# Routing and scattering each 96-token chunk inside a batch-major attention loop, with one region of rows per expert

## The reference, cut to what matters

```python
def _moe_ref(x, w_gate, w1, w2, capacity):
    logits = x @ w_gate
    expert_idx = np.argmax(logits, axis=1)
...
    for i in range(N):
        e = expert_idx[i]
        if counts[e] < capacity:
            disp[e, counts[e]] = x[i]
            pos[i] = counts[e]
            counts[e] += 1
            keep[i] = True
    h = np.maximum(np.einsum('ecd,edf->ecf', disp, w1), 0.0)
    y = np.einsum('ecf,efd->ecd', h, w2)
...
    for i in range(N):
        if keep[i]:
            out[i] = gate_w[i] * y[expert_idx[i], pos[i]]
def _moe2_ref(x, w_a, w_b, w_out):
    a = x @ w_a
    b = x @ w_b
    return (a * b @ w_out).astype(np.float32)
```

## Time and profile before

| what | value |
|---|---|
| runs | 677.47, 677.79, 680.08 us; median 677.79 us |
| span of the profiled execution, first to last instruction | 679.2 us |
| its own device time | not given apart from its span; its span lies inside the three times |
| TensorE busy | 511.9 us, 75% |
| VectorE busy | 381.5 us, 56% |
| ScalarE busy | 263.2 us, 39% |
| POOL busy | 39.9 us, 6% |
| mean granted TensorE clock | 0.958 of full speed |
| DMA | 60.5 MB, 89 GB/s on average |

### The profile page before, as it was taken

How to read it: one execution, slowest core, us unless ns; L and a number is a source line. 1 busy time by engine, 2 the same in 40 slices (tenths; PEclk the granted TensorE clock), 3 DMA queues, 4 the chain that set the end, 5 groups by cost and what they waited for, 6 DMA issues and landing times.

```text
span 679.2 us, 9804 instructions
## 1 busy us (share of the span) xinstructions
PE 511.9 (75%) x3682; PEld 475.1 (70%) x3683; DVE 381.5 (56%) x751; ACT 263.2 (39%) x483; POOL 39.9 (6%) x47
## 2 busy tenths in 40 slices
PE   0000001688999994088999999899999999999995
PEld 0000001578999993088999999888888888888884
DVE  3999999997555546245777777644432222221220
ACT  6930514881111113134766667534433121131121
POOL 1000000000000002750000000000002000020002
PEclk9999999789999996588999999989999999999998
DMA  8960001341121105665455554422101000010001
GB/s 335 297 64 0 0 0 69 140 122 37 36 55 36 37 1 204 215 201 198 132 198 185 184 183 140 141 70 92 49 0 47 1 0 1 0 47 0 0 0 46
DMA packets 47955, 60.49 MB, mean 89 GB/s; under 512 B 25072, under 2 KB 40944, under 8 KB 47408
## 3 DMA queue, kind: packets, MB, share of 16 engines
q1 hardware_dynamic: 46384, 55.28, 26.5%
q0 software_dynamic: 1536, 4.73, 2.0%
HBM read 50.55 MB, written 9.45 MB: 88 GB/s over the span
## 4 chain that ended last, share of the span: by engine, by line
PE 70%; DVE 19%; ACT 3%; issue 3%; POOL 3%; DMA 2%; SPq 0%; ACTq 0%; DVEq 0%; POOLq 0%
PE bank L1065 23%; PE bank L1052 10%; PE bank L931 10%; PE bank L895 10%; PE bank L580 4%; PE bank L488 3%; PE bank L559 3%; DVE region L313 3%; DVE XN L310 2%; POOL sorted_x L714 2%; PE bank L584 2%; DVE XN L311 2%; PE bank L595 1%; DVE XN L350 1%; DVE QN L350 1%
## 5 line engine op out<-in xcount | busy, mean ns | idle before, releaser
L1083 DVE TENSOR_TENSOR ga<-ga,bank 128x512 f32<-128x512 f32 x36 | 24.8, 688 | 137.4 <-PE bank L1065 137.4
L366 PE MATMUL bank<-ident,ends 128*96 128x128 f32 x4 | 1.1, 420 | 100.5 <-DVE ends L329 100.5
L366 PEld LDWEIGHTS bank<-ident,ends 128*96 128x96 f32 x4 | 0.6, 187 | 100.1 <-issue 100.1
L931 PE MATMUL bank<-hh,w2h 128*128 128x256 f32 x192 | 54.4, 283 | 1.8 <-ACT w1h L736 1.8
L895 PE MATMUL bank<-xh,w1h 128*128 x192 | 54.4, 284 | 0.0
L931 PE MATMUL bank<-hh,w2l 128*128 128x256 f32 x192 | 54.2, 283 | 0.0
L931 PE MATMUL bank<-hl,w2h 128*128 128x256 f32 x192 | 54.2, 282 | 0.0
L895 PE MATMUL bank<-xh,w1l 128*128 x192 | 53.7, 280 | 0.0
L895 PE MATMUL bank<-xl,w1h 128*128 x192 | 53.6, 279 | 0.0
L1085 ACT ACTIVATE gh<-ga 128x512 fp32r<-128x512 f32 x36 | 22.8, 632 | 79.1 <-DVE ga L1083 79.1
L1081 ACT ACTIVATE ga<-bank 128x512 f32<-128x512 f32 x36 | 21.5, 597 | 80.7 <-PE bank L1065 80.7
(11 more groups left out here) (175 smaller groups left out, 1373.5 us busy)
## 6 DMA issues: line engine op xcount, KB each, us to landing
raw<-w SPq DMA_DIRECT2D x16, 1536.0 KB, 7.1
x_rows<-XN SPq DMA_DIRECT2D x4, 1152.0 KB, 4.2
XN<-x_rows SPq DMA_DIRECT2D x14, 288.0 KB, 3.1
region<-k SPq DMA_DIRECT2D x4, 576.0 KB, 12.6
region<-q SPq DMA_DIRECT2D x4, 576.0 KB, 16.2
V<-v SPq DMA_DIRECT2D x1, 2304.0 KB, 29.3
raw<-wa SPq DMA_DIRECT2D x6, 384.0 KB, 3.2
raw<-wb SPq DMA_DIRECT2D x6, 384.0 KB, 3.9
```

What stands on the lines that cost most here:

```text
L931: m = nc.tensor.matmul(bank[YB0 + c][:, 0:cols], wx[:, f, c * P:(c + 1) * P], xx[:, f, 0:cols], start=f == 0 and i == 0, stop=f == NF - 1 ...
L1083: m = dve.done(tt(ga[f % 2][:], ga[f % 2][:], bb[:, 0:TT], ALU.mult))
```

## The change

The units are now ordered by batch, then piece, then group, and the host hands q, k, v, a_re and a_im over with the two batches swapped, so that the batch worked first is the first half of the tokens. Chunk t of 96 tokens is complete after units 2t and 2t+1, in token order. The diff below is in the order of the streams: the zero fill behind the input loads, ScalarE's wait in front of the copy to eT (L369), three operations more in `set_up`, the loop's new helpers and where it calls them (`choose` ahead of `scores(n + 1)`; `ranks` and `place_chunk` behind u and ahead of y; the wait ahead of the product with `swap`), what follows the loop, and the experts. Each chunk is routed inside the loop: its choice of expert (`choose`), its rank by two or three small products (`ranks`), its slots and its scatter (`place_chunk`). The slot is e x 1536 + rank, in a `sorted_x` with a region of rows for each expert; regions are filled with zeros up to the capacity at the start. w1 and w2 of expert 0 are loaded half way through the loop into memory that QT of the first batch left. Rows are read for one expert at a time (384 rows), and turned and split inside `outputs` of the expert before. Gate and index no longer travel with the rows: after `hidden(0)` VectorE works out the final place of each token and its gate, and POOL scatters pairs (gate, index) to a small DRAM table `place_rows`, which is read back during expert 6.

```diff
+            zero = eT[:, :, :].rearrange("p i q -> p (i q)")[:, 0:DM]
+            m_zrow = pool.done(g.memset(zero, 0.0))
+            sp.wait_ge(pool.sem, m_zrow[1])
+            for e in range(E):
+                sp.dma_start(sorted_x[e, 0:CAP, :].rearrange("(i p) c -> p i c", p=P),
+                             zero.unsqueeze(1).broadcast_to([P, XT_N, DM])).then_inc(s_zero, 16)
...
+            ss.wait_ge(s_zero, 16 * E)
+            m_eT = act.done(ss.activation(eT[0:C2], bank[7][0:C2, :].rearrange("p (i q) -> p i q", i=4), ACT.Copy))
...
+                dve.done(vv.tensor_copy(trib[:], tri[:]))
+                dve.done(vv.tensor_scalar(baseb[:], basef[0:L], ident[0:L, 0:1], None, ALU.mult))
+                m_const.append(dve.done(vv.tensor_copy(mark[:, :, 1], tok)))
...
-            units = [(j, gr) for j in range(NC) for gr in range(NU)]
+            GB = NU // B
+            units = [(j, (B - 1 - b) * GB + gr) for b in range(B) for j in range(NC) for gr in range(GB)]
...
+            def choose(t):
+                dve.wait(m_lgs[t])
+                m = dve.done(vv.tensor_reduce(out=mx[:, t:t + 1], in_=lg(t), axis=AXX, op=ALU.max))
+                dve.wait(m)
+                m = dve.done(vv.scalar_tensor_tensor(out=eqp, in0=lg(t), scalar=mx[:, t:t + 1], in1=pri,
+                                                     op0=ALU.is_equal, op1=ALU.mult))
+                m_read_lg = m
+                dve.wait(m)
+                m = dve.done(vv.tensor_reduce(out=best[:, t:t + 1], in_=eqp, axis=AXX, op=ALU.max))
+                dve.wait(m)
+                m_oh[t] = dve.done(vv.tensor_scalar(ohb[:, t, :], eqp, best[:, t:t + 1], None, ALU.is_equal))
+                act.wait(m_read_lg)
+                m_lx.append(act.done(ss.activation(lgs[:, t, :], lg(t), ACT.Copy)))
+            def ranks(t, m_jd_last):
+                pe.wait(m_oh[t], *m_const)
+                if m_jd_last:
+                    pe.wait(m_jd_last)
+                nc.tensor.matmul(rk[0:L], onesb[:, 0:L], baseb[:], start=True, stop=False)
+                if t:
+                    pe.wait(m_so[t - 1])
+                    nc.tensor.matmul(rk[0:L], onesb[:, 0:L], so[:, t - 1, :], start=False, stop=False)
+                m_rk[t] = pe.done(nc.tensor.matmul(rk[0:L], trib[:], ohb[:, t, :], start=False, stop=True))
+            def place_chunk(t):
+                if t:
+                    dve.wait(m_so[t - 1], m_oh[t])
+                    m_so[t] = dve.done(tt(so[:, t, :], so[:, t - 1, :], ohb[:, t, :], ALU.add))
+                else:
+                    dve.wait(m_oh[0])
+                    m_so[0] = dve.done(vv.tensor_copy(so[:, 0, :], ohb[:, 0, :]))
+                dve.wait(m_rk[t])
+                m_tk[t] = dve.done(tt(sel[:, t, :], rk[0:L], ohb[:, t, :], ALU.mult))
+                dve.wait(m_tk[t])
+                m = dve.done(vv.tensor_reduce(out=rank[:, t:t + 1], in_=sel[:, t, :], axis=AXX, op=ALU.add))
+                dve.wait(m)
+                m_slot[t] = dve.done(vv.tensor_copy(sloti[:, t:t + 1], rank[:, t:t + 1]))
+                pool.wait(m_slot[t], m_yx[(t + 1) * GB - 1])
+                if t == 0:
+                    g.wait_ge(s_zero, 16 * E)
+                g.indirect_dma_start(out=sorted_x.rearrange("e n c -> (e n) c"),
+                                     out_offset=bass.IndirectOffsetOnAxis(ap=sloti[:, t:t + 1], axis=0),
+                                     in_=X[:, t, :], in_offset=None).then_inc(s_sc, 16)
...
+                if n % GB == 1 and done >= 0 and n > GB:
+                    choose(done)
...
+                if n == NUNIT // 2:
+                    sp.wait_ge(pe.sem, m_y[n - 1][1])
+                    for s_, x, y in ((s_w1, w1[0].rearrange("(c p) f -> p c f", p=P), raw_0[0]),
+                                     (s_w2, w2[0].rearrange("(f p) n -> p f n", p=P), raw_0[1])):
+                        sp.dma_start(y.rearrange("p (c f) -> p c f", f=x.shape[-1]), x).then_inc(s_, 16)
...
+                if n % GB == 1 and done >= 0 and n > GB:
+                    ranks(done, m_turned_z)
+                    place_chunk(done)
...
+                        if m_tk:
+                            pe.wait(m_tk[max(m_tk)])
                         m_j = pe.done(nc.tensor.matmul(bank[7][0:C2, 0:YB * D], swap[:], zm[0], start=True, stop=True))
...
+            sp.wait_ge(s_sc, 16 * TAU)
+            load_rows(0)
...
+        for i in range(4):
+            nc.tensor.matmul(bank[i][:, 0:CAP], ident[:], ident[:].unsqueeze(1).broadcast_to([P, XT_N, P]),
+                             start=True, stop=True)
...
+        m_t0 = [turn_tile(i, bank[4 + i]) for i in range(XT_N)]
+        for i in range(XT_N):
+            m_x0 = split_tile(i, bank[4 + i], m_t0[i])
+        sp.wait_ge(pe.sem, m_t0[-1][1])
+        load_rows(1)
...
+                    i = f // 2
+                    if f % 2 and i < tiles:
+                        if i:
+                            pe.wait(m_x[i - 1])
+                        else:
+                            nc.tensor.wait_ge(s_row, (e + 2) * 16)
...
-                w1_marks[0] = [split(*piece1(f)) for f in range(NF)]
+                w1_marks[0] = []
+                for f in range(NF):
+                    w1_marks[0].append(split(*piece1(f)))
+                    if f % 2 and f // 2 < tiles:
+                        assert split_tile(f // 2, bank[7], m_t[f // 2]) == m_x[f // 2]
+                row_marks[0] = (m_t[-1], m_x[-1])
...
+        m_w2 = hidden(0, m_x0, True)
...
+        def chosen(out_, x):
+            D_(tt(sel, ohb[:], over_t(x), ALU.mult))
+            D_(vv.tensor_reduce(out=out_, in_=sel, axis=AXX, op=ALU.add))
...
+        m = D_(tt(ex, lgs, over_e(mx), ALU.subtract))
+        act.wait(m)
+        m_exp = act.done(ss.activation(ex, ex, ACT.Exp))
+        D_(tt(over, tot, kept, ALU.subtract))
+        D_(vv.tensor_tensor_scan(out=cumo, data0=one8, data1=over, initial=cumk[:, E - 1:E],
+                                 op0=ALU.mult, op1=ALU.add))
+        D_(tt(frs, cumo, over, ALU.subtract))
+        D_(vv.scalar_tensor_tensor(out=frs, in0=frs, scalar=-float(CAP), in1=fst, op0=ALU.add,
+                                   op1=ALU.subtract))
+        chosen(comp, basef)
+        D_(tt(rank, rank, comp, ALU.subtract))
+        chosen(comp, frs)
+        D_(vv.scalar_tensor_tensor(out=comp, in0=rank, scalar=float(CAP), in1=comp, op0=ALU.is_ge, op1=ALU.mult))
+        D_(tt(rank, rank, comp, ALU.add))
+        chosen(comp, fst)
+        D_(tt(rank, rank, comp, ALU.add))
+        dve.done(vv.tensor_copy(compi[:], rank))
+        dve.wait(m_exp)
+        D_(vv.tensor_reduce(out=den, in_=ex, axis=AXX, op=ALU.add))
+        D_(vv.tensor_scalar(den, den, 1e-9, None, ALU.add))
+        D_(vv.reciprocal(den, den))
+        m_mark = D_(tt(mark[:, :, 0], den, den, ALU.mult))
+        s_mark, s_placed = sem("s_mark"), sem("s_placed")
+        pool.wait(m_mark)
+        for t in range(TAU):
+            g.indirect_dma_start(out=place_rows[:, :],
+                                 out_offset=bass.IndirectOffsetOnAxis(ap=compi[:, t:t + 1], axis=0),
+                                 in_=mark[:, t, :], in_offset=None).then_inc(s_mark, 16)
...
         def trip(e, more=True):
             outputs(e, False)
+            sp_wait(row_marks[0][0])
+            if more:
+                load_rows(e + 2)
```

More of the change, by code:

```diff
@@ L496, in scores @@
                     SC[r], maski, bank[2 + r][0:L, 0:YB * L].rearrange("p (i c) -> p i c", i=YB)))
+            loaded = [n for n in range(0, len(units), XB) if units[n][0] < NC - 1]
             def load_x(i):
-                j, gr = units[i * XB]
-                if i >= len(XS):
-                    sp.wait_ge(pe.sem, m_u[(i - len(XS) + 1) * XB - 1][1])
-                sp.dma_start(XS[i % len(XS)],
+                j, gr = units[loaded[i]]
+                if i >= NXS:
+                    sp.wait_ge(pe.sem, m_u[loaded[i - NXS] + XB - 1][1])
+                sp.dma_start(XS[i % NXS],
@@ L535, in build @@
+            s_w1, s_w2 = sem("s_w1"), sem("s_w2")
             NUNIT = len(units)
-            NX = (NC - 1) * NU // XB
+            NX = len(loaded)
             sp.wait_ge(s_xrows, 16 * SL)
             sp.wait_ge(pe.sem, m_turn[len(late_q0) + len(late_x) - 1][1])
-            for i in range(len(XS)):
+            for i in range(NXS):
                 load_x(i)
             scores(0)
+            m_added = m_turned_z = None
             for n in range(NUNIT + 2):
+                done, turned, x_at = chunk(n) - 1, None, None
+                if n % GB == 1 and done >= 0 and n > GB:
+                    choose(done)
@@ L543, in build @@
                 if n + 1 < NUNIT:
                     scores(n + 1)
-                turned = None
-                if n - 1 in ready:
+                if n % GB == 0 and n:
+                    turned = chunk(n - 1)
                     pe.wait(m_yx[n - 1])
-                    turned = turn_rows(ready[n - 1], n)
```

(53 more changed lines are left out.)

362 lines of the change are left out of this document (147 added, 215 removed).

## The result

The kernel after the change takes 682.26 us, median of four runs (681.49 to 685.29); the kernel before, run beside it, takes 677.95 us, median of four (677.47 to 680.08). The ratio is 1.0071 with a 95% interval of 1.0044 to 1.0099: slower by 0.4% to 1.0%. The forecast was 663.2 us, 656 to 671, and faster; it was wrong, in size and in sign.

A forecast was written before the change was run, and what follows sets the result against it. TensorE was taken to bound the loop and the experts, with a 52.4 us chain between (258.5 to 310.85 us). Terms 0.5 + 1.8 + 2.0 - 26.2 + 1.4 + 5.9 = -14.6 gave a median of 663.2 us, range 656 to 671.

The forecast's parts named there:

- Points 1 and 2: Start of kernel: zero fill behind the loads, price 0; three more small VectorE operations in set_up, +0.5 us.
- Points 3 and 4: Attention loop: rank products for 15 chunks, +1.8 us; TensorE's waits at three uncovered places, +2.0 us (bounds 0.5 and 5).
- D: Rival, loop: routing chain between VectorE and TensorE becomes each chunk's bound; slower, 682 us; chance 0.05.
- E: Rival, loop: POOL is held, scatters pile up and the last stands behind 15 others; 683 us; chance 0.04.
- Point 5: Last y to outputs(0): 26.2 us instead of 52.4, of which 14.5 until hidden(0) starts; -26.2 us.
- Point 6: outputs(0): a 2.1 us wait behind VectorE's small operations replaces the low clock; 11.5 for 10.08 us, +1.4.
- Point 7: outputs(1) to (6): three tiles in each, 18 x 0.33 us on a full TensorE, +5.9 us.
- Point 8: Experts: 16 small scatters on idle POOL and a 12 KB read in expert 6, long before use; price 0.
- The offset to the median: Whole sum: made against the profiled span, 679.2 us, taken as 1.4 above the 677.8 median, difference carried over.
- A: Rival: clock stays at 1.2 GHz for all of hidden(0) and falls again in outputs(0); 669 us; chance 0.10.
- B: Rival, expert trips: w1 loads start later behind rows and land late, up to 1.5 us in six trips; 672; chance 0.08.
- C: Rival, loop: POOL's scatter holds VectorE as well, 15 x 0.92 = 13.8 us; 677 us; chance 0.05.

The follow-up runs named there:

- late: The kernel after, with POOL holding its 16 pair scatters until w1 of expert 5 has landed: 685.89 us, ratio 1.011 against the kernel before.
- the wide rows: The kernel after with pair scatters held until w1 of expert 5 landed, plus 16 scatters of 512-byte rows at their old place: 701.1 us, one run.

## Why the prediction was right in its stages and wrong in its result

- **Points 1 and 2, zero fill and `set_up`.** Right. The fill stands nowhere in the chain, and the three operations of `set_up` take 0.34 us there for the 0.5.
- **Points 3 and 4, rank products and waits in the loop.** Right: a chunk takes 7.02 us (mask copies at 240.61 and 247.63) for the 6.85 of the earlier trace rows, and the whole loop is 4.1 us longer where the two terms said 3.8. The chain goes through `choose` at two of the three places named, 0.95 us each (from 206.34 and from 259.64), for the 2.0 of point 4; the other 2.2 us lie with the products, for the 1.8 of point 3. D is out, and E too: the last scatter goes alone at 267.01.
- **Point 5, last y to outputs(0).** From the last y, at 262.3, to the first product of hidden(0), at 276.77, there are 14.5 us, as the sum said; in it the scatter took 2.55 and the row read 3.74 for the 4.0 taken. By the Trainium skill, DMA: Bandwidth & Descriptors, section on the anatomy of one DMA, an estimate for the read was 3.4; the measured 3.74 lies about halfway between it and the 4.0. The page fits that rule to transfers that GpSimd issues, and SP issues this one. (The 772 KB of the old read are counted in 1024 bytes and the 590 of the new one in 1000; in the same unit they are 790 and 590.) hidden(0) took 10.36 for 9.96 (8.46 and the clock's 1.5). Its end to outputs(0) did not stay 1.74 but took 3.05, and the waits of this kernel name why:

```profile
PE bank L895 <- DVE route L964: 3.1, 1, 3.1
```

  `outputs` finds the marks of hl by counting back from the end of VectorE's stream (`dve.n - 2 * NF + 2 * f + 2`; with NF = 8 and f = 0 that is 14 back). With 20 operations put behind hidden(0) this is the sixth of them, L964, which has nothing to do with hl. The prediction had these operations lie beside TensorE's work here. With them moved ahead of hidden(0) the gap is 0.
- **Point 6, outputs(0).** 11.6 us (290.18 to 301.8) for the predicted 11.5, but half by luck. The forecast let a wait of 2.1 for the first tile's split *replace* the low clock. The low clock came: the first 18 products took 3.92 us for the usual 2.14, and the row in it is

```profile
292.00:294.00 2.00, 2.00 (x12) 2.00 (x12) 1.64 (x8) 0.00 (x0) 0.00 (x0) 0.56 1.07 399
```

  So TensorE had its first four groups and a tile behind it at 296.55 and waited only 0.13 us, to 296.68. VectorE's operations took what the sum said (xl was ready 6.4 us after outputs(0) began, for 6.7), and the clock filled the time of the wait. By these numbers either of the two alone would have given about the same end, and the chain of the kernel without scatters does go through VectorE here (xl at 296.17); with VectorE's operations moved, and the gap ahead of outputs(0) with them, both are gone, and it is 9.5.
- **Point 7, tiles in outputs.** The chain of the kernel after has 18 products in 2.14 us and three of a tile in 0.33 throughout: as predicted. Every hidden also takes 8.62 for 8.46, 1.0 us in six, which the sum did not have.
- **Point 8, places and gates.** The step that failed, and the one that turned the sign. It asked whether the result of the 16 scatters comes in time, and priced at 0 what they do to others while they run. outputs(0) begins 20.7 us earlier than before (290.18 for 310.85), and all that follows takes 22.1 us longer (390.4 for 368.4, each to its span's end). Of these 22.1 the stretch from outputs(0)'s end to hidden(1)'s end is 14.6 (23.07 for the 8.46 of the earlier trace rows). outputs(0) adds 1.5, outputs(1) to (6) 6.9 (5.9 of it the tiles, the rest their own products), hidden(2) to (7) 1.0, and the bilinear layer, which the change doesn't touch, gives back 2.0 (236.0 for 238.0).
- **The offset to the median.** Without the burst the kernel takes 669.5, still 6 us over the forecast. 3.2 of these are the steps above: the span is then 667.8 for the predicted 664.6. The rest is the yardstick. The profiled execution of before was taken as 1.4 us above the median, its span against a time; but in every later result the time of a run is its span and 1.7 to 1.9 us. So that execution took some 681, 3 us above the median of 678, 2 us of it in the bilinear layer. A sum made against an execution above the median, in stages that the change leaves alone, carries that over.
- **Rivals.** A: the clock is 0.50 at the start of hidden(0), as forecast, and back at 0.97 from 280 on, 3.2 us after the first product. The second half of A, a low clock in outputs(0) again, did come (0.59 and 0.56 from 290 to 294, point 6), and it is 0.50 again in the stall. B: no wait of ScalarE for raw stands in the trips outside the stall. C: no operation of VectorE in the loop grew, 0.35 us for the state operations and 0.57 for the mask copies. Its mechanism exists all the same, in another place: a clear of POOL held a cast for 3.91 us. D's sum was off besides: with a chain 1.2 us too long it gives 1.4 us more than before, 0.2% and not half a per cent. The test "a time over 674 would say that the argument of point 4 is wrong" was itself wrong, for point 4 held at 682.

## What to carry to other kernels

A burst of DMAs on POOL has a price for all engines, even where nobody waits for its data: do not issue 16 without a wait; wait after every fourth, or tie each to an event that comes every few microseconds. Price a hidden step twice, once for when its result is due and once for what it holds while it runs, and look for marks that are found by counting back before putting operations into a stream. Before summing against one profiled execution, see whether it is typical in the stages that stay the same.

## What the runs showed of the hardware that was not expected

- **A queue of POOL's transfers starves the other engines.** Sixteen indirect scatters back to back cost 12.8 (the kernel after), 13.5 (the kernel before) and 17.0 us (late, span 684.8 less 667.8), and two such bursts 31.5; sixteen plain ones cost about 4, four at a time nothing. In the stall of the kernel after, from 311.9 to 315.5, TensorE started a weight load or a product every 0.70 us, and SP's issue of a load took 0.70 us where the earlier trace rows has 0.39. The profile lists a DMA queue of the kind "instruction". From 290 to 320 us the kernel after has its row first, the kernel without scatters second:

```profile
q8 instruction: 2, 0.03, 1.0%
```

```profile
q8 instruction: 2, 0.03, 0.4%
```

  The two packets took 1.0% of 16 engines' 30 us, 2.4 us each, for 1.0 us each without scatters. That would fit instructions that come through the same DMA engines and stand behind POOL's transfers there. It is argued, not shown, and other kernels speak against it: with the wide rows, hidden(1) is stretched as much, and the two packets take 0.4% as without scatters; and while TensorE stands for 11.39 us in their second burst (390.40 to 401.79), no packet of an instruction queue is recorded. No run changed that queue alone. By what path the burst holds the engines up stays open.
- **A clear of POOL locks out some operations of VectorE and not others.** The cast, with one input in SBUF, waited 3.91 us; products and differences with two inputs beside the first clear did not. The Trainium skill, SBUF — State Buffer, section "SBUF: two separate sides", says that the port pair of VectorE and GpSimd is an exclusive lock, which VectorE needs in a two-port mode, and with two SBUF inputs only against a GpSimd operation that reads SBUF. The trace agrees, since a clear reads nothing: the second half is shown by the two-input operations, and the first as far as that the cast was held; that it ran in a two-port mode the trace does not say. Rival C had taken the shorter form of the rule.
